# Retention layer and two expert layers: another order of TensorE's work in the attention chunk, constants in groups, w2's first conversion moved

## What is computed

```python
# 1: linear attention, B=4, H=8, S=768, D=64; gamma by head
state = gamma * state + k[t] (outer) v[t]
y[t] = q[t] @ state / sqrt(D)
# 2: x = y as (3072, 512); each token goes to the expert of its largest gate logit
logits = x @ w_gate;  e = argmax(logits)
out = softmax(logits)[e] * sigmoid(x @ w_output_gate)[e] * (relu(x @ w1[e]) @ w2[e])
# 3: soft experts: softmax over tokens of out @ phi makes 32 slots, 4 for each
# of 8 experts; their outputs are mixed back by the softmax over slots
```

## Time and profile before

| | |
|---|---|
| median of 3 runs | 582.3 us |
| the profiled execution | 582.56 us, its span 580.6 us |
| PE busy | 534.2 us (92%) |
| DVE, ACT, POOL busy | 250.7, 194.9, 139.8 us |
| attention, first scores to last xT | 4.3 to 125.7 us |
| routing, to the first expert product | 125.7 to 152.1 us |
| experts and the rest | 152.1 to 580.6 us |
| share of DMA engines busy in attention | 0.44 to 1.02 by windows of 8 us up to 120 us |

### The profile page before, as it was taken

The page is one execution under the profiler, slowest core; times in us unless marked ns, Lnnn a source line. Parts: engine busy times, 40 slices in busy tenths (PEclk is TensorE's granted clock), DMA queues, the critical chain, the costliest instruction groups (busy, mean ns, idle before and its releaser), DMA issues.

```text
span 580.6 us, 10956 instructions
## 1 busy us (share of the span) xinstructions
PE 534.2 (92%) x4503; PEld 448.6 (77%) x4503; DVE 250.7 (43%) x425; ACT 194.9 (34%) x367; POOL 139.8 (24%) x145
## 2 busy tenths in 40 slices
PE   4999999962899999999999999999999999969992
PEld 3777777741699899899899899999989989932551
DVE  2446666457224263353363354354344434033432
ACT  2223333220124264262362453354344444120142
POOL 2314141302602044034025025024123023021000
PEclk9999999995599999999999999999999999978996
DMA  8899988710309408707616624234242145988988
GB/s 319 296 347 363 330 333 282 271 61 17 107 1 327 169 5 256 238 9 242 217 42 210 213 78 161 73 122 146 62 149 94 53 153 192 379 298 320 423 300 292
DMA packets 47460, 115.42 MB, mean 199 GB/s; under 512 B 5733, under 2 KB 16382, under 8 KB 45886
## 3 DMA queue, kind: packets, MB, share of 16 engines
q1 hardware_dynamic: 38334, 99.86, 48.5%
q0 software_dynamic: 5200, 7.95, 5.0%
q10 hardware_dynamic: 3888, 7.08, 3.2%
HBM read 101.03 MB, written 13.82 MB: 198 GB/s over the span
## 4 chain that ended last, share of the span: by engine, by line
PE 80%; issue 7%; DMA 4%; DVE 4%; POOL 3%; ACT 1%; SPq 0%; POOLq 0%; DVEq 0%; ACTq 0%
PE bank L1268 18%; PE bank L1269 18%; PE bank L1270 17%; PE bank L1473 3%; PE ybank L1245 3%; PE bank L1213 2%; DMA out<-orow 2%; POOL k_decayed L541 2%; PE ybank L1339 2%; PE ybank L1363 2%; PE bank L1281 2%; PE bank L1188 1%; PE bank L1442 1%; PE bank L1226 1%; PE bank L1327 1%
## 5 line engine op out<-in xcount | busy, mean ns | idle before, releaser
L1268 PE MATMUL bank<-xT_hi,w_hi 128*128 128x432 f32 x256 | 97.9, 382 | 1.0 <-DVE xT_lo L947 1.0
L1268 PE MATMUL bank<-hT_hi,w_hi 128*128 128x432 f32 x256 | 94.1, 368 | 0.0
L1269 PE MATMUL bank<-xT_lo,w_hi 128*128 128x432 f32 x256 | 93.0, 363 | 0.0
L1270 PE MATMUL bank<-xT_hi,w_lo 128*128 128x432 f32 x256 | 92.7, 362 | 0.0
L1269 PE MATMUL bank<-hT_lo,w_hi 128*128 128x432 f32 x256 | 92.0, 359 | 0.0
L1270 PE MATMUL bank<-hT_hi,w_lo 128*128 128x432 f32 x256 | 91.9, 359 | 0.0
L952 DVE SCALAR_TENSOR_TENSOR hT_lo<-bank,hT_hi 128x432 fp32r<-128x432 f32 x64 | 38.9, 608 | 116.2 <-ACT hT_hi L682 114.4
L562 POOL DMA_INDIRECT slot_logits<-lcur,logit_row_of_row x32 | 32.2, 1005 | 152.6 <-DVE lcur L961 145.2
L682 ACT ACTIVATE hT_hi<-bank 128x432 fp32r<-128x432 f32 x64 | 34.0, 531 | 103.4 <-PE bank L1270 102.9
L1268 PEld LDWEIGHTS bank<-xT_hi,w_hi 128*128 128x128 f32 x256 | 49.0, 191 | 9.8 <-issue 6.3
L686 ACT ACTIVATE yT<-bank 128x432 f32<-128x432 f32 x32 | 17.0, 531 | 107.0 <-PE bank L1270 107.0
(11 more groups left out here) (180 smaller groups left out, 694.4 us busy)
## 6 DMA issues: line engine op xcount, KB each, us to landing
w_raw<-in_w SPq DMA_DIRECT2D x64, 512.0 KB, 5.9
v_units<-in_v SPq DMA_DIRECT2D x20, 1024.0 KB, 10.3
qk<-in_qk SPq DMA_DIRECT2D x24, 512.0 KB, 4.2
kv<-in_kv SPq DMA_DIRECT2D x24, 512.0 KB, 5.9
v_units<-in_v SPq DMA_DIRECT2D x4, 2048.0 KB, 16.5
x_rows<-xrow ACTq DMA_DIRECT2D x27, 256.0 KB, 3.1
out<-orow SPq DMA_DIRECT2D x12, 512.0 KB, 5.8
v<-in_v SPq DMA_DIRECT2D x2, 2048.0 KB, 10.8
```

The costliest lines, as they stand in the source:

```text
L1268: pe.matmul(out, wh, xh, start=first_, stop=False)
L1269: pe.matmul(out, wh, xl, start=False, stop=False)
L1270: return pe.matmul(out, wl, xh, start=False, stop=last_)
```

## The change

- **PE's order in a chunk** becomes scores, q-state, gates, turns, gate sum, kv product, both half products. The waits for xT and state of the chunk before (`s_y`, `s_S`) stand ahead of q-state, those for v and the decayed k ahead of the kv product. The gate sum stands directly behind the turns, the two half products directly behind the kv product.
- **Constants** come in three transfers: what mask and decays need, then (after `wg`) identity and slot sum, and the rest after the loads of three chunks. `wg` and `phi` hold their columns once (64 KB each). ACT converts the bf16 constants after the last chunk instead of at the start. The two stores of zeros to x_rows (256 KB each) and the memsets before them fall away; two one-column ACT instructions raise the same semaphores.
- **Weights**: one w1 piece is loaded after each of rounds 0 to 3; ACT converts it after chunk c = 3 of batch 0, 1, 2, 3, DVE in chunk c = 5, before it waits for the output. The four w2 pieces are loaded after the last round and converted by ACT and DVE among the tiles of expert 0, as in the other experts.

```diff
...
@@ -420,15 +427,17 @@
                 if isinstance(i, int) and i == 0:
-                    sp.dma_start(const[:, :], const_h).then_inc(s_const, 16)
+                    sp.dma_start(const[:, 0:N_FIRST], const_h[:, 0:N_FIRST]).then_inc(s_const, 16)
+                    sp.dma_start(wg[:, :, :], wg_h).then_inc(s_wg, 16)
+                    sp.dma_start(const[:, N_FIRST:N_TURN], const_h[:, N_FIRST:N_TURN]).then_inc(s_turn, 16)
                 sp.dma_start(kv[par][:, :, :], kv_h[i]).then_inc(s_kv[par], 16)
                 if isinstance(i, int) and i == 0:
                     sp.dma_start(yscale[:, :, :], yscale_h).then_inc(s_ysc, 16)
-                    sp.dma_start(wg[:, :, :], wg_h).then_inc(s_wg, 16)
             for par in range(NB):
                 load(par, par)
             sp.dma_start(phi[:, :, :], phi_h).then_inc(s_phi, 16)
+            sp.dma_start(const[:, N_TURN:], const_h[:, N_TURN:]).then_inc(s_rest, 16)
...
@@ -454,10 +463,11 @@
                 load_round(r_)
-                for p in range(r_ % 2 * 2, r_ % 2 * 2 + 2):
-                    (load_w1, load_w2)[r_ // 2](0, p)
+                load_w1(0, r_)
             with sp.Fori(4, T // NB - 1) as r_:
                 load_round(r_)
+            for p in range(NP):
+                load_w2(0, p)
             for par in range(2):
...
@@ -518,8 +528,6 @@
-            for par in range(2):
-                pool.memset(xrow[par][:, :], 0.0)
             pool.memset(acc[:, :], 0.0)
...
@@ -621,10 +629,9 @@
             for par in range(2):
-                act.dma_start(x_d[par * P:(par + 1) * P, :], xrow[par][:, :]).then_inc(s_xst[par], 16)
+                act.activation(xrow[par][:, 0:1], stat[:, 7:8], ACT.Copy).then_inc(s_xst[par], 16)
             act.activation(stat[:, 7:8], stat[:, 7:8], ACT.Copy).then_inc(s_gev, 1)
             act.wait_ge(s_const, 16)
-            act.activation(const16[:, :], const[:, C_16:C_16 + N_16], ACT.Copy).then_inc(s_c16, 1)
             act.activation(stat[:, 6:7], stat[:, 6:7], ACT.Copy).then_inc(s_lg, 1)
...
@@ -651,12 +658,14 @@
                     keep(bt * CH + c, c % 2, bt * (CH // 2) + c // 2 + 1)
-                    if c in (1, 3):
-                        for kind in range(2):
-                            with act.If(bt == kind + 1):
-                                for p in range(c // 2 * 2, c // 2 * 2 + 2):
-                                    (w1_high, w2_high)[kind](0, p)
-
+                    if c == 3:
+                        for p in range(NP):
+                            with act.If(bt == p):
+                                w1_high(0, p)
+
+            act.activation(const16[:, 2 * P + T:], const[:, C_IOTA:C_IOTA + P], ACT.Copy)
+            act.wait_ge(s_rest, 16)
+            act.activation(const16[:, 0:2 * P + T], const[:, C_TRI:C_TRI + 2 * P + T], ACT.Copy).then_inc(s_c16, 1)
             act.wait_ge(s_gt, T + 1)
...
@@ -711,20 +720,20 @@
                     rows_keep(i - 1, 0)
-                    w2_high(i, 0)
+                w2_high(i, 0)
                 h_high(i, 3)
                 if i > 0:
                     rows_keep(i - 1, 1)
-                    w2_high(i, 1)
+                w2_high(i, 1)
                 h_high(i, 4)
                 if i > 0:
                     slot_exp(i - 1)
                     rows_keep(i - 1, 2)
...
@@ -821,7 +830,6 @@
             dve.wait_ge(s_mask, 1)
-            dve.wait_ge(s_ysc, 16)
             with dve.Fori(0, BATCH) as bt:
...
@@ -839,11 +847,12 @@
                         last.then_inc(s_S, 1)
-                    if c in (2, 4):
-                        for kind in range(2):
-                            with dve.If(bt == kind + 1):
-                                for p in range(c - 2, c):
-                                    (w1_low, w2_low)[kind](0, p)
+                    if c == CH - 1:
+                        dve.wait_ge(s_hi1, bt + 1)
+                        at = bass.ds(bt * PIECE, PIECE)
+                        dve.tensor_tensor(w1_lo[:, at], w1_raw[:, at], w1_hi[:, at].bitcast(F32), ALU.subtract).then_inc(s_lo1, 1)
+                    if c == 0:
+                        dve.wait_ge(s_ysc, 16)
                     dve.wait_ge(s_av, i + 1)
...
@@ -995,22 +1004,21 @@
                 h_low(i, 2)
-                if i > 0:
-                    w2_low(i, 0)
+                w2_low(i, 0)
                 h_low(i, 3)
                 if i > 0:
                     slot_max(i - 1)
-                    w2_low(i, 1)
+                w2_low(i, 1)
                 h_low(i, 4)
                 if i > 0:
                     max_keep(i - 1)
...
@@ -1176,13 +1184,13 @@
-                pe.wait_ge(s_const, 16)
+                pe.wait_ge(s_turn, 16)
                 pe.wait_ge(s_wg, 16)
                 pe.wait_ge(s_y, i + 1)
                 pe.wait_ge(s_gev, i + 1)
                 for k in range(KT):
                     g_ = slice(k * SLOTS, (k + 1) * SLOTS)
-                    mm = pe.matmul(bank[4][g_, 0:P], wg[:, k, g_], xT[:, k, :], start=True, stop=True)
+                    mm = pe.matmul(bank[4][g_, 0:P], wg[:, k, :], xT[:, k, :], start=True, stop=True)
                 mm.then_inc(s_gt, 1)
...
@@ -1205,40 +1213,33 @@
                     for a_ in range(PAIRS):
-                        if c == CH - 1 and a_ == PAIRS - 1:
-                            pe.wait_ge(s_y, i + 1)
-                            pe.wait_ge(s_S, bt * (CH - 1) + c + 1)
                         for n in range(2):
                             h_ = slice(n * HD, (n + 1) * HD)
                             mm = pe.matmul(bank[n][:, a_ * P:(a_ + 1) * P], qk[par][h_, 1, a_, :], qk[par][h_, 0, a_, :],
                                            start=True, stop=True)
                             if a_ == PAIRS - 1:
                                 mm.then_inc(s_sc, 1)
+                    if c > 0:
+                        pe.wait_ge(s_y, i + 1)
+                        pe.wait_ge(s_S, bt * (CH - 1) + c + 1)
+                        pe.sem_inc(s_alone_pe, 1)
+                        for a_ in range(PAIRS):
+                            for n in range(2):
+                                h_ = slice(n * HD, (n + 1) * HD)
+                                pe.matmul(y_at(a_, n), state[h_, a_, :], qk[par][h_, 0, a_, :],
+                                          start=(a_ < 2), stop=False, skip_group_check=True)
+                    gates(i)
+                    gate_sum(i)
+                    pe.wait_ge(s_kv[par], 16 * n_par)
                     if c < CH - 1:
-                        pe.wait_ge(s_kv[par], 16 * n_par)
-                        if c > 0:
-                            pe.wait_ge(s_y, i + 1)
-                            pe.wait_ge(s_S, bt * (CH - 1) + c + 1)
                         pe.wait_ge(s_kd, bt * (CH - 1) + c + 1)
                         for a_ in range(PAIRS):
                             for n in range(2):
                                 e_ = slice((2 * a_ + n) * HD, (2 * a_ + n + 1) * HD)
                                 mm = pe.matmul(bank[7][n * HD:(n + 1) * HD, a_ * HD:(a_ + 1) * HD], kdec[:, e_], kv[par][:, 1, e_],
                                                start=True, stop=True)
-                    if c > 0:
-                        for a_ in range(PAIRS):
-                            for n in range(2):
-                                h_ = slice(n * HD, (n + 1) * HD)
-                                mm = pe.matmul(y_at(a_, n), state[h_, a_, :], qk[par][h_, 0, a_, :],
-                                               start=(a_ < 2), stop=False, skip_group_check=True)
-                    if c < CH - 1:
                         mm.then_inc(s_kvd, 1)
-                    else:
-                        pe.wait_ge(s_kv[par], 16 * n_par)
-                    gates(i)
                     for n in range(2):
-                        if n == 1:
-                            gate_sum(i)
                         pe.wait_ge(s_m, 2 * i + n + 1)
...
```

More of the change, by code:

```diff
@@ L52 @@
 BIG = 1e30
-C_ID, C_SUM, C_TRI, C_ONE, C_IOTA = 0, 128, 256, 384, 512
-C_J = C_IOTA + P
-C_16, N_16 = C_TRI, 3 * P + T
-C_P = C_J + T
-C_W8 = C_P + 1
-C_RST = C_W8 + NE
-C_KD = C_RST + NE * T
+C_IOTA = 0
+C_P = C_IOTA + P
+C_KD = C_P + 1
 C_SD = C_KD + HEADS
 C_GS = C_SD + PAIRS
-C_DUMP = C_GS + HEADS
+N_FIRST = C_GS + HEADS
+C_ID = N_FIRST
+C_SUM = C_ID + P
+N_TURN = C_SUM + P
+C_TRI = N_TURN
+C_ONE = C_TRI + P
+C_J = C_ONE + P
+C_W8 = C_J + T
+C_RST = C_W8 + NE
+C_DUMP = C_RST + NE * T
 C_N = C_DUMP + NCH * NS
+N_16 = 3 * P + T
 ROUTE = ["mx", "eq", "cand", "mw", "hot", "hsum", "lgs", "og8", "t4", "og", "rk", "k", "qi", "qf", "far", "r", "t",
@@ L151, in program @@
         const = put("const", [C_N])
-        phi = put("phi", [KT, P])
+        phi = put("phi", [KT, SLOTS])
         idx = put("token_of_row", [TW + XW], I32)
@@ L204, in program @@
         const16 = put("const16", [N_16], BF16, at=r)
-        wg = put("wg", [KT, P], at=r)
+        wg = put("wg", [KT, SLOTS], at=r)
```

(26 more changed lines are left out.)

## The result

| | before | after |
|---|---|---|
| median of 4 runs each | 582.1 us (581.19 to 582.79) | 567.97 us (566.18 to 570.3) |
| profiled execution, time and span | 582.56, 580.6 us | 566.18, 564.3 us |
| start of chunk 1 | 14.82 | 10.50 |
| chunk c = 1 to 4, c = 5, c = 0, undisturbed | 4.84, 4.50, 4.24 | 4.42, 3.96, 3.82 |
| last xT | 124.96 | 110.27 |

The ratio is 0.9756 (95% interval 0.9736 to 0.9775): 14.1 us faster, inside the range and 1.2 above the forecast of 566.8. The profiled execution is the fastest of the four after the change. Two executions among the experiments ran far slower at a lower granted clock and are left out of all medians and ratios: one of the eight with PE's old order (870.11 us) and one of the nine of the kernel before beside the last two experiments (679.38 us).

The account below looks back on a forecast made before the run. PE's order was taken to bound the attention stage, with time lost at shape changes and loads second. 582.56 - 13.9 - 3.8 + 1.5 + 0.7 = 567.1, or 566.8 us against the median; range 562.5 to 572.5.

Parts of the forecast that it names:

- chunks 1 to 23, without new waits: Attention chunks on PE, 110.1 us before, were to take 96.2 with fewer shape changes: 13.9 us saved (9 to 18).
- other new waits: Waits for xT and state, gate parts, decayed k and DVE's w1 piece: together 0.7 us lost (0 to 3).
- Half products and kv product merged: On PE in each full chunk, two merges saving 0.15 each: 0.30 us (0.18 to 0.46).
- Gate sum behind the turns: On PE in each chunk, both groups take 0.80 in place of 1.00, saving 0.20 us (0.10 to 0.23).
- Chunks with two weight pieces: Chunks where DVE, busy with two weight pieces in a row, comes late: 1.9 us go with single pieces.
- The start: Before chunk 1: less loaded ahead of kv, PE's idle time filled; chunk 1 starts at 11.0, saving 3.8 us (2.4 to 4.5).
- The w1 piece: Batch 0, chunk 4: gate sum waits behind ACT's conversion of the first piece, 1.5 us lost once (0 to 3).
- third rival: Gate sum outruns ACT's gate parts: each of 24 chunks waits 0.1 to 0.3 us, 569 to 574 us; chance 0.08.
- second rival: Loads come late: at 345 GB/s chunks can't be shorter than 4.31 while w1 is loaded, 570.5 us; chance 0.13.
- fourth: State loop (kv product, state, decayed state, decayed k) becomes the bound with POOL stretched by DVE: slower, 584 us; chance 0.04.
- w2's conversion in expert 0: ACT and DVE convert w2 among expert 0's hidden tiles, covered by idle time: nothing lost, 0 to 2 us allowed.
- The later stages: Stages after the last xT: the routing stage, with its lower clock, only moves earlier; no change in length counted.

Follow-up runs that it names:

- the last two experiments: Changed kernel with ACT's w1 piece one chunk later and ACT issuing wg and second constants, 566.67 us; on top, gate sum moving 16 columns, not 128, 564.59 us.

## Why the prediction came out

The mechanism held, and the total came out 1.2 off because several errors balanced. That it came so close is in part luck: 1.6 us of the gain in the profiled execution come from stages that the forecast had at nothing, and they make up for a term that was 1.9 too large. In the order of its steps, for the profiled execution:

| term | predicted | measured |
|---|---|---|
| chunks 1 to 23, without new waits | -13.9 | -12.0 |
| start of chunk 1 | -3.8 | -4.3 |
| first w1 piece | +1.5 | +1.6 |
| other new waits | +0.7 | 0.0 |
| from the last xT on | 0 | -1.6 |
| sum of the spans | -15.5 | -16.3 |

- **Half products and kv product merged: right.** Predicted 0.30 of a chunk, measured 0.31 (0.11 and 0.20). The 0.15 a merge, taken from the middle of two bounds, held in the mean of the two.
- **Gate sum behind the turns: mis-sized.** Predicted 0.20, measured 0.11, in every chunk: 23 x 0.09 is 2 us, and it is the whole miss of the first term. The turns fell by 0.09 as the earlier trace rows showed. Two steps failed. "Two records at 0.49/4 = 0.12 and one gap of 0.10" gives 0.34 for the gate sum, which took 0.39; and "the refill of the gate sum's own start goes too" took off another 0.03 that did not go. Turns and gate sum take 0.50 + 0.39 = 0.89, not 0.80. (The bound beside it, "two records cost 0.09", is 0.09 for one record: 0.59 - 0.41 = 0.18 for two.) A likely cause is the load of the gate sum's weights (PEld), which are the gate parts, the very data it waits for:

```profile
17.10 0.28 ACT L648 ACTIVATE gate_parts<-bank 128x128 f32<-128x128 f32 x1 [2.39 <-PE bank L1193]
17.43 0.30 PEld L1203 LDWEIGHTS bank<-const,gate_parts 128*128 128x128 f32 x2
```

ACT's copy ends at 17.38 and the load starts 0.05 later. The records of the turns start 0.11 apart, each together with the load of the next one's weights; the gate sum's second record starts 0.18 after its first. With an eighth of the columns the sum still takes 0.30, which fits. But in the kernel before, where the copy was done 0.76 ahead of the gate sum (17.90, and 18.66 in the earlier trace rows), the sum took 0.41 with a change of shape at both its ends. This order with early gate parts was not run, so the share of the load is argued and not shown.

- **Chunks with two weight pieces: right.** The 1.9 us are gone. With the old order the single pieces cure them too; with the new order and two pieces they make chunks 1.8 to 3.9 us too long, four times. The step of the text was right, but the whole plan hung on it more than it said: 11.7 us, not 1.9.
- **The start: right for half the reason.** Chunk 1 starts at 10.50, within 10.3 to 12.4 and at its fast end. The text let kv land at 6.3 to 7.3 and the decayed k be ready near 8; it landed at 7.9 instead of 8.27 and the decayed k was ready at 9.0. What gained was the work in PE's idle 3.00 us and the full pace afterwards, for which the range had both ends. Both terms of its landing were mis-sized, by one profile of each kernel: the smaller volume was put at 2.0 us and the two transfers more ahead of kv at 1.0. With those two issued by ACT, kv is issued at 1.65 as before the change, and POOL starts at 6.52, 1.75 earlier than before. With them in front, kv is issued at 2.59 and POOL starts at 7.91, 1.4 later than that.
- **The w1 piece: right in size, too narrow in its bounds.** From the end of chunk 2 the text said: landed at 6.9, converted at 8.0, gate sum at 8.4. Measured from 19.34: 7.3, 8.3 and 8.5. Its bounds, 0 to 3, left out the clock: other profiles show waits of 2.79 and 3.07 here, and what follows them at half pace made 4.5 and 5.3 us of them over chunks 4 and 5 (the 0.6 of DVE's piece taken off the second).
- **Other new waits: none.** The margin of 0.08 between ACT's gate parts and the gate sum is there in the chunk above (17.38 to 17.46), and no row shows a wait outside chunk 4 (third rival: did not occur as told; if the late load of the weights is the cause of the 0.05 above, that is this rival on a smaller scale). Nor did the loads come late, at a DMA share of 0.98 and 0.99 (second rival), nor the state loop bind (fourth). Even with POOL stretched to 2.02 behind two weight pieces, in the kernel with the order alone, PE waited for DVE's xT and not for the decayed k. That two pieces in a row undo the gain by way of xT stood in no rival.
- **w2's conversion in expert 0: right, at nothing.** ACT's rows between hidden tiles, which answer to the earlier trace rows, keep the pitch of 2.37 with the piece between them and 0.90 us idle left of 1.84:

```profile
146.89 0.53 ACT L691 ACTIVATE hT_hi<-bank 128x432 fp32r<-128x432 f32 x1 [1.84 <-PE bank L1271]
147.32 1.05 ACT L643 ACTIVATE w_hi<-w_raw 128x1024 fp32r<-128x1024 f32 x1
149.26 0.53 ACT L691 ACTIVATE hT_hi<-bank 128x432 fp32r<-128x432 f32 x1 [0.90 <-PE bank L1271]
```

- **The later stages: not foreseen.** The text let them only move earlier. They also became 1.6 us shorter in all: routing 0.5 longer (27.6 from the last xT to the first expert product, against 27.1), the experts 1.1 shorter, 0.9 of it in expert 0 (43.7 against 44.7), and 1.0 shorter behind the experts (70.8 against 71.8). The products of the tail, first before and then after the change:

```profile
517.21 1.94 PE L1363 MATMUL ybank<-y_rows,pT 108*32 108x128 f32 x32 [0.80 <-ACT y_rows L694]
```

```profile
501.94 1.08 PE L1364 MATMUL ybank<-y_rows,pT 108*32 108x128 f32 x32 [0.85 <-ACT y_rows L703]
```

The same 32 instructions after about the same wait, once at half and once at full pace: the granted clock there is 0.54 before (516 to 518) and 0.81 after (502 to 504). In expert 0 the clock is back 3.6 us after its first product instead of 5.7. No instruction of these stages explains it: the last two kernels, with ACT's piece and loads moved, have the slow tail again (1.94 for this group) and an expert 0 that is 1.0 longer (44.8 and 44.7), with the same code there. So about 2 us in the total come and go with when the clock falls and returns.

**What stays open.** The four executions after the change span 4.1 us, those before 1.6. The first w1 piece, whose wait was between 0.3 and 3.1 us over the profiles, fits as a cause; but the kernel in which nothing waits for it still spreads over 3.4 us (565.63 to 569.02). Open too are the stops of PE without a releaser and what makes the gate sum's 0.39.

## What to carry to other kernels

Where PE is never idle, count its changes of shape: equal shapes next to each other saved 0.1 to 0.2 us for each break that went. The gate sum, whose weights are the awaited data, itself fell by only 0.02. A new order on one engine moves due times on all the others: list what each engine does ahead of the result that is now wanted earlier (here wg's load and DVE's weight pieces) and move that first; here the order alone gained nothing. A one-off wait of 3 us on PE cost 1.6 and 1.7 times its length here, so take the long ones away before many short ones.

## What the runs showed of the hardware that was not expected

- Two changes of shape on PE around a small product cost 0.21 us, the product itself 0.11. The Trainium skill (TensorEngine Tiling (Array Packing), Key Properties) says that a switch of mode drains TensorE. These runs agree that it costs time, and put a number to it.
- PE's clock after a stop, in the rows: after 1.42 and 1.83 us the granted clock stayed at 1.00. After 1.97 it was 0.50 between 32 and 34. After 2.79 it was 0.50 between 35 and 37, and the first two groups behind the wait still had the full pace. After 3.07 the first product behind the wait was slow already. Yet in the kernel with the order alone it stayed at 1.00 after a wait of 2.15 (50 to 56) and fell to 0.52 after one of 2.12 (84 to 86): the length of the wait alone does not tell. The lower level is 1.2 GHz of 2.4.
- In chunk 0 the granted clock reads 1.00 while the scores take 2.08 us instead of 1.16. At the very start the pace shows only in the lengths.
- The same tail ran at half or at full pace by nothing that its own code does, worth 1 us.
